# Expert products of a mixture-of-experts kernel: the high part of the weights streams both parts of its operand in one matmul

## What is computed

```python
# 1. attention with decay, block 64, q, k, v of (2, 8, 768, 64)  ->  x of (1536, 512)
# 2. mixture of experts: N, D, E, F = 1536, 512, 8, 1024
logits = x @ w_gate
expert_idx = argmax(logits, axis=1); gate_w = softmax(logits)[expert_idx]
for e in range(E):
    xe = x[expert_idx == e]
    h = maximum(xe @ w1[e], 0.0)
    out[expert_idx == e] = gate_w * (h @ w2[e])
# 3. dense: 512 -> 2048 -> 512
h = x @ w_in
y = (h - tanh(h)) @ w_out
```

## Time and profile before

| | us |
|---|---|
| median of three executions | 549.39 (548.83 to 557.4) |
| the profiled execution, its own time | 552.58 |
| its span | 550.8 |
| granted TensorE clock, mean over the span | 0.98 |
| TensorE busy, share of the span | 93% |
| experts, from the first product of the second expert to the end of the last x2_h | 118.3 to 276.2 |

### The profile page before, as it was taken

How to read it: one execution, slowest core, us unless ns; L and a number is a source line. 1 busy time by engine, 2 the same in 40 slices (tenths; PEclk the granted TensorE clock), 3 DMA queues, 4 the chain that set the end, 5 groups by cost and what they waited for, 6 DMA issues and landing times.

```text
span 550.8 us, 10819 instructions
## 1 busy us (share of the span) xinstructions
PE 511.6 (93%) x3948; PEld 454.6 (83%) x3949; DVE 364.0 (66%) x496; ACT 257.4 (47%) x467; POOL 317.8 (58%) x258
## 2 busy tenths in 40 slices
PE   2999848799999999999989999999999999999994
PEld 2899748799999999999968888888888888888883
DVE  2433275856455365454469999998998784998781
ACT  0222216556566566566454545545443434443431
POOL 4566235634454454444449889985855553875553
PEclk9999959999999999999999999999999999999998
DMA  7988615656757757667280000000100000100002
GB/s 223 374 292 281 225 31 175 205 169 208 234 175 227 230 196 222 195 210 232 90 302 6 2 0 1 0 1 20 58 0 0 1 1 1 58 20 1 1 0 77
DMA packets 33450, 65.35 MB, mean 119 GB/s; under 512 B 3680, under 2 KB 8800, under 8 KB 33376
## 3 DMA queue, kind: packets, MB, share of 16 engines
q1 hardware_dynamic: 31488, 58.49, 32.7%
q0 software_dynamic: 1920, 6.29, 3.5%
HBM read 58.22 MB, written 6.55 MB: 118 GB/s over the span
## 4 chain that ended last, share of the span: by engine, by line
PE 85%; DMA 5%; DVE 3%; issue 3%; ACT 2%; SPq 1%; POOL 1%; ACTq 0%; DVEq 0%; POOLq 0%
PE bank L306 25%; PE bank L308 24%; PE bank L307 24%; DMA wst<-in_w_dram 3%; PE bank L1075 3%; PE bank L1052 2%; PE bank L1063 2%; PE bank L1097 1%; PE bank L1087 1%; PE bank L1161 1%; PE bank L1104 1%; DVE x_sorted L952 1%; DMA w_gate_sb<-in_w_gate_dram 1%; POOL out_dram L621 1%; DMA x_sorted<-token_rows,tokid 1%
## 5 line engine op out<-in xcount | busy, mean ns | idle before, releaser
L579 POOL TENSOR_TENSOR w_l<-wst,w_h 128x512 fp32r<-128x512 f32 x64 | 84.4, 1319 | 107.4 <-ACT w_h L684 107.3
L629 POOL TENSOR_SCALAR big<-h_sq 128x512 uint8<-128x512 f32 x48 | 79.8, 1663 | 38.3 <-ACT h_sq L768 38.0
L642 POOL TENSOR_TENSOR g_l<-g,g_h 128x512 fp32r<-128x512 f32 x48 | 63.6, 1325 | 46.5 <-ACT g_h L778 46.5
L306 PE MATMUL bank<-wo_h,g_h 128*128 128x512 f32 x192 | 75.4, 393 | 0.0
L308 PE MATMUL bank<-wo_l,g_h 128*128 128x512 f32 x192 | 75.1, 391 | 0.0
L307 PE MATMUL bank<-wo_h,g_l 128*128 128x512 f32 x192 | 74.6, 389 | 0.0
L308 PE MATMUL bank<-x_l,win_h 128*128 128x512 f32 x188 | 74.4, 395 | 0.0
L306 PE MATMUL bank<-x_h,win_h 128*128 128x512 f32 x188 | 73.9, 393 | 0.0
L306 PE MATMUL bank<-xs_h,w_h 128*128 (+1 forms) x256 | 71.3, 279 | 2.6 <-DVE xs_l L958 1.4
L307 PE MATMUL bank<-x_h,win_l 128*128 128x512 f32 x188 | 73.7, 392 | 0.0
L306 PE MATMUL bank<-h_h,w_h 128*128 128x232 f32 x256 | 71.6, 280 | 1.7 <-DVE h_l L942 1.6
(11 more groups left out here) (145 smaller groups left out, 1094.7 us busy)
## 6 DMA issues: line engine op xcount, KB each, us to landing
wst<-in_w_dram SPq DMA_DIRECT2D x128, 256.0 KB, 3.0
qk_in<-in_qk_t_dram SPq DMA_DIRECT2D x12, 512.0 KB, 5.5
kv_in<-in_kv_dram SPq DMA_DIRECT2D x12, 512.0 KB, 5.2
win<-in_w_in_dram SPq DMA_DIRECT2D x8, 512.0 KB, 4.7
wo<-in_w_out_dram SPq DMA_DIRECT2D x8, 512.0 KB, 8.6
token_rows<-x_sb SPq DMA_DIRECT2D x12, 256.0 KB, 3.5
mask<-decay_powers SPq DMA_DIRECT2D x4, 128.0 KB, 3.3
decay_powers<-powers SPq DMA_DIRECT2D x1, 256.0 KB, 2.9
```

The costliest lines, as they stand in the source:

```text
L306: pe.matmul(dst, lh, rh, start=start, stop=False, skip_group_check=True)
L579: pool.tensor_tensor(w2_l[:, j % STG], wst2[:, j % STG], w2_h[:, j % 2].bitcast(F32), ALU.subtract).then_inc(w2l_ready, 1)
L629: pool.tensor_scalar(big[:, f % 2], h_sq[:, f % 2], T * T, None, ALU.is_ge).then_inc(big_ready, 1)
L642: pool.tensor_tensor(g_l[:, f % 2], g[:, f % 2], g_h[:, f % 2].bitcast(F32), ALU.subtract).then_inc(gl_ready, 1)
```

## The change

Each product makes two matmuls where it had three. The high weight part streams both parts of the operand (464 columns) into the two halves of one bank; the low weight part streams the high part of the operand (232 columns) into the first half. A bank so holds two partial results, and they are added when the bank is read out:

- `hidden`: DVE first adds the two halves (a reduction over an axis of two, from PSUM, to h_plain in SBUF, L966 of the new file); ACT takes relu of that to the high part (L700); DVE makes the low part (L969), now from two operands in SBUF. Hidden banks alternate between 0 and 1.
- y takes four banks (4 to 7) of two halves each, and there is one such set. After an expert's last product ACT copies the second halves to `rows` in two pieces (`y_in`, L728), DVE adds the first halves to them (L996) giving x2, at unit 0 of the next expert; at unit 1 `y_out` makes x2_h and x2_l from x2, now in SBUF. The second product of unit 0 of the next expert waits for the two sums.
- The turned tiles use banks 2 and 3; xs_h and xs_l become one tensor xs.

```diff
+        def both(b):
+            return bank[:, b, 0:2 * WIN].rearrange("p (a t) -> p a t", a=2)
...
+        def y_bank(half, side):
+
+            return bank[:, 4 + 2 * half:6 + 2 * half, side * WIN:(side + 1) * WIN]
+
+        def two(pe, b, lh, ll, r, start, stop):
+
+            pe.matmul(both(b), lh, r, start=start, stop=False, skip_group_check=True)
+            return pe.matmul(both(b)[:, 0], ll, r[:, 0], start=False, stop=stop, skip_group_check=True)
...
 # ACT
             def hidden(j, unit):
-                act.wait_ge(first_done, unit + 1)
-                act.activation(h_h[:, j % 2], bank[:, j % 4, 0:WIN], ACT.Relu).then_inc(hh_ready, 1)
+                act.wait_ge(hsum_ready, unit + 1)
+                act.activation(h_parts[:, j % 2, 0], h_plain[:, j % 2, 1], ACT.Relu).then_inc(hh_ready, 1)
...
+            def y_in(expert_no, off):
+
+                for half in range(2):
+                    if half:
+                        act.wait_ge(second_done, JT * expert_no)
+                    else:
+                        act.wait_ge(y_half_done, expert_no)
+                    act.copy(rows[:, 2 * half:2 * half + 2, bass.ds(off, WIN)], y_bank(half, 1)).then_inc(y_side_ready, 1)
+
+            def y_out(expert_no, off):
+                act.wait_ge(y_sum_ready, 2 * expert_no)
+                act.copy(x2_h[:, :, bass.ds(off, WIN)], x2[:, :, bass.ds(off, WIN)]).then_inc(y_high_ready, 1)
...
                     hidden(j, unit)
+                    if j == 0 and not first:
+                        y_in(e, off)
...
 # DVE
             def hidden(j, unit):
+                dve.wait_ge(first_done, unit + 1)
+                dve.tensor_reduce(h_plain[:, j % 2, 1], both(j % 2).rearrange("p a t -> p t a"), AX.X,
+                                  ALU.add).then_inc(hsum_ready, 1)
                 dve.wait_ge(hh_ready, unit + 1)
-                dve.scalar_tensor_tensor(h_l[:, j % 2], bank[:, j % 4, 0:WIN], 0.0, h_h[:, j % 2].bitcast(F32),
+                dve.scalar_tensor_tensor(h_parts[:, j % 2, 1], h_plain[:, j % 2, 1], 0.0, h_parts[:, j % 2, 0].bitcast(F32),
                                          ALU.max, ALU.subtract).then_inc(hl_ready, 1)
...
+            def y_in(expert_no, off):
+
+                for half in range(2):
+                    sl = slice(2 * half, 2 * half + 2)
+                    dve.wait_ge(y_side_ready, 2 * expert_no - 1 + half)
+                    dve.tensor_tensor(x2[:, sl, bass.ds(off, WIN)], y_bank(half, 0), rows[:, sl, bass.ds(off, WIN)],
+                                      ALU.add).then_inc(y_sum_ready, 1)
...
 # PE
-                    i = three(pe, bank[:, j % 4, 0:WIN], w1_h[:, j % 2, k, :], w1_l[:, j % STG, k, :],
-                              xs_h[:, k, bass.ds(off, WIN)], xs_l[:, k, bass.ds(off, WIN)], k == 0, k == KT - 1)
+                    i = two(pe, j % 2, w1_h[:, j % 2, k, :], w1_l[:, j % STG, k, :], xs[:, k, :, bass.ds(off, WIN)],
+                            k == 0, k == KT - 1)
...
+                    if j == 0 and k % 2 == 0 and summed is not None:
+
+                        pe.wait_ge(y_sum_ready, summed + k // 2)
                     sl = slice(k * P, (k + 1) * P)
-                    i = three(pe, psYs[side][:, k], w2_h[:, j % 2, sl], w2_l[:, j % STG, sl], h_h[:, j % 2], h_l[:, j % 2],
-                              j == 0 and k % 2 == 0, j == JT - 1)
+                    i = two(pe, 4 + k, w2_h[:, j % 2, sl], w2_l[:, j % STG, sl], h_parts[:, j % 2], j == 0, j == JT - 1)
+                    if j == JT - 1 and k == 1:
+                        i.then_inc(y_half_done, 1)
```

More of the change, by code:

```diff
@@ L118, in decay_attention_moe_kernel @@
         rows, x2_h = twice("rows", "x2_h", [P, KT, PAD])
[L119 removed]
+        x2, x2_l = twice("x2", "x2_l", [P, KT, PAD])
         win_h = sb("win_h", [P, KT, F2], F32R)
@@ L180, in decay_attention_moe_kernel @@
         expert_no = sb("expert_no", [1, E, OV], at=experts_mem)
-        h_h = sb("h_h", [P, 2, WIN], F32R, at=experts_mem)
-        h_l = sb("h_l", [P, 2, WIN], F32R, at=experts_mem)
+        h_plain, h_parts = twice("h_plain", "h_parts", [P, 2, 2, WIN], at=experts_mem)
         experts_mem.close()
@@ L594, in _, with expert @@
                 gather(t)
-            def expert(e, side, first=False, last=False):
+            def expert(e, first=False, last=False):
                 for j in range(JT):
@@ L734, in expert @@
                     if j == 1 and not first:
-                        y_out(JT * e, off, 1 - side, e - 1)
+                        y_out(e, off)
                     if j == (JT - 1 if first else 3):
@@ L983, in expert @@
                     if j == 1 and not first:
-                        y_out(e, off, 1 - side)
+                        y_out(e, off)
                     if j == (JT - 1 if first else 3):
@@ L1195, in expert @@
                         first_product(offset(e + 1), 0, JT * e + JT)
-                    if j == 0 and not first:
-                        ge(pe, y_low_ready, e - 1)
                     if first:
                         turn(LATER[j])
-                    second_product(j, JT * e + j, side)
+                    second_product(j, JT * e + j, None if first else 2 * e - 1)
             pe.wait_ge(ov_step, 2)
```

55 lines of the change are left out of this document (31 added, 24 removed).

## The result

The changed kernel takes 573.07 us (median of 4, 572.3 to 574.2), the kernel before 549.11 (median of 4, 547.0 to 557.4): a ratio of 1.0423, interval 1.038 to 1.0466. It is slower, on the side forecast and inside the range, 5.4 us above the point. Of one kernel's executions, those over 1.5% above its fastest (here the 557.4) are left out of the ratios and intervals of this document. The profiled execution took 572.8 us, 20.2 above the profiled one of before, where I had worked out 18.3.

What follows compares the result with a forecast made beforehand. Experts looked bound by TensorE, but DVE and ACT were already on the path where x2_h and x2_l are made. 9 + 4.9 + 3.7 + 0.5 = +18; 549.4 + 18.3 = 567.7 us, range 557 to 580.

Steps and rivals of the forecast that it cites:

- The two waits: In each expert TensorE idles for h_parts at units 2 and 4, behind x2_l and win_l: 1.85 and 1.3 us.
- a plain unit: A unit without output or split work: 2.58 us instead of 2.68, the hidden part's round trip hidden.
- The lock of the ports: VectorE with two SBUF inputs and GpSimd exclude each other; h_l can be held, at worst 1 us more per round trip.
- Five experts: The long stretch between second expert and last: +1.8 us an expert, +9 in all.
- first boundary: First change of expert, split of w_in still in front: 27.0 us against 22.1, +4.9.
- first expert: Expert with the turned tiles: slower steps of 3.7 to 4.1 us, offset by the incident's going; net +0.5 us.
- incident: First expert before: a scaling of 4.62 us behind POOL instructions, then a lower clock; 3.3 us lost, taken as gone.
- The last expert: Seven units, both waits, and 1.25 us more behind the last matmul: 28.2 against 24.5, +3.7.
- The dense stage: Stage after the experts: forecast as untouched by the change.
- the slow reduction: Rival: reading pairs 232 columns apart, the reduction takes 1.12 us and DVE sets the pace; 590 us, chance 0.08.
- TensorE did not stay the bound: Rival that TensorE stays the bound, waits as before: 540 to 544 us, below 538 with faster 464-column matmuls; chance 0.09.
- The incident returns: Rival: POOL's instructions again in a row as DVE scales in the first expert; 572 to 573 us, chance 0.13.

Runs made afterwards that it cites:

- no_sum: Changed kernel without DVE's reduction in the hidden part, relu and low part reading the first half of the bank alone: 548.79 us, 0.9942 of the kernel before.
- late_lows: Changed kernel with all of x2_l and win_l made behind the last expert, the reduction kept: 558.7 us (one execution), an expert 20.93 us.
- pieces: Changed kernel with x2_h, x2_l, win_h and win_l made in four pieces each, spread over units, behind the reduction: 549.42 us, 0.9981 of the kernel before.
- sum_first: Changed kernel with the reductions of units 2 and 4 put ahead of x2_l and win_l: 571.18 us, 1.0393 of the kernel before.
- before_pieces: Kernel before, three matmuls kept, with x2 copies and win splits in four pieces each: 548.34 us, 0.9952 of the kernel before.
- pieces_hoist: As pieces, plus in the first expert the next unit's reduction ahead of the turned tiles' low parts: 547.22 us, 0.9954 of the kernel before.
- sum_first_split: As sum_first, with POOL making w2_l in two instructions of 256 columns: 569.2 us, 1.0305 of the kernel before.
- sum_first_u2: Changed kernel with only the reduction of unit 2 put ahead of x2_l: 571.48 us, 1.0387 of the kernel before.
- pieces_hoist_split: As pieces_hoist, with POOL making w2_l in two instructions of 256 columns: 548.5 us, 0.9976 of the kernel before.

## Why the prediction was right, and where it was off

**Right in the mechanism.** DVE between product and relu, and behind it the low part of x2 and the split of w_in: `no_sum` gives back all of the slowdown, and `late_lows` and `pieces` show that the reduction costs nothing where no long step stands ahead of it. The two waits measured 1.65 and 1.32 in the expert shown, 1.54 to 1.89 and 1.27 to 1.31 in the other experts of the long stretch, as far as they have a row, 1.54 and 1.55 in the second expert (forecast 1.85 and 1.3), a plain unit 2.57 (2.58), the reduction 0.63 (0.64), a 464-column matmul 0.21. An expert took 24.29 against 24.1. The lock of the ports, which I let fall on h_l, met x2_l instead: 1.45 us where I had 1.12.

**The terms.** Five experts +10.1 for +9; first boundary +5.4 for +4.9, with TensorE waiting 2.35 for the sums as worked out (2.4) and 0.32 for the last hidden part (1.0); first expert −0.3 for +0.5, the steps between turns 3.65 to 4.47 where I had 3.7 to 4.1, and no incident. It is gone in this trace and in those of `sum_first`, `late_lows`, `pieces` and `before_pieces`, but since the kernel before itself has it in different sizes, and `pieces_hoist` has it again, my reason (POOL is not in a row any more in that order) was not tested.

Some sums do not come out as written. The four terms make 18.1, and 18.3 went into the time. The first boundary takes the two waits at 1.3 and 1.3 where the walk had 1.85 and 1.3. For the last expert, 1.8 an expert and 1.25 behind it make 3.05, not 3.7. For the first, 4.6 and 0.6 less 3.3 is +1.9, less the 1.8 for the clock too +0.1; neither is +0.5. None of this is over 1.5 us.

**The last expert, +3.7 forecast, +4.7 to x2_h ready.** I counted a copy, one sum and x2_h, 2.1 us, behind the last matmul. The chain has 3.2 from 292.97, where half of y is there, or some 2.6 from the end of the last matmul at about 293.5: both sums follow the copy, 0.61 and 0.65 one behind the other, and the handovers come to 0.35. Two more waits of TensorE were not in the forecast: 0.36 for the second sum of the expert before, and 0.39 for the last unit's own round trip (290.40 to 292.05), which has no next first product to hide it.

**The dense stage, "untouched" in the forecast, cost +1.5.** TensorE was idle 2.69 us ahead of it; then 12 matmuls ran at a granted clock of 0.69 and the first two behind them took 0.43, not 0.23. That the hole could cost clock as well I had seen in the incident of the earlier trace rows and not applied here. Whether that is the change's doing stays open: before, a hole of 2.41 us was followed by a full clock in the first trace, while the second one, behind a hole of 2.12, had 4.47 us for the same 12 matmuls. The gap of 1.35 us that did not return, −1.2, was in no term either; that the two nearly cancel is luck.

**What put the point 5.4 us low is mostly the base.** I said "I add the difference to the median": 549.4 + 18.3. But the difference was made against a trace that holds the incident at 4.62 us, and I counted its going as a gain, while the median execution lies 3.2 under that trace. The base should have been the profiled execution: 552.6 + 18.3 = 570.9, within 2.2 of the result. So 3.2 of the 5.4 us come from the base, 1.9 from the terms, and 0.3 from a median of the changed kernel that lies above its own trace. The median of before looks low too: 59 later executions of that kernel, in three groups, have medians of 550.0 to 551.5. The traces show the incident changing from run to run; that it is what lifts that one execution above the median is argued, not shown.

**Of the rivals,** the slow reduction fell (464 elements, read in pairs 232 apart, 0.63 on the line of steps that read PSUM side by side). TensorE did not stay the bound. "The incident returns" gave a number near the result (572 to 573) by the wrong mechanism: in the trace of 572.8 us every scaling took 0.48 or 0.49.

## What to carry to other kernels

A shorter instruction on the busiest engine gains only what the others leave it: here a pair that saved 0.1 us a unit put one more step on DVE between two products, and each long step queued on DVE ahead of it became a wait of 1.3 to 1.9 us. Before making such a change, look at what stands in the queue ahead of the new step; cut it into pieces that fit the place where the engine waits anyway, or spread them over the units. Such pieces alone, without the pair, gave the kernel before the same 0.5%.

Taking a result from PSUM into SBUF first can lengthen the step that reads it next: x2_l went from 1.12 to 1.45 us beside POOL.

If a trace holds a stall that may not be in every execution, keep that trace's own time as the base for a forecast that takes the stall away, and take a second trace of the same kernel first.

## What the runs showed of the hardware

- DVE's h_parts, two inputs in SBUF, took 0.40 alone and 1.50 beside one POOL instruction of 1.26 us (`sum_first`); 0.91 beside POOL instructions half as wide. Halving POOL's instructions cut the single hold, from 1.10 to 0.52, but not the sum of the holds in a unit (`sum_first_split`).
- The same subtraction of 128x928, x2_l, took 1.12 in 8 of 8 cases with one input in PSUM (`before`), and with both in SBUF 1.44 to 1.46 in the seven cases beside POOL, 1.13 in the one without (the changed kernel).
- The same scaling of 128x512 on DVE took 0.48, 1.72, 1.81, 3.92, 4.62 or 4.80 us in different traces; 1.81 and 4.62 are the same kernel. The one of 4.62 us, 102.42 to 107.04, ran beside POOL instructions that stood end to end from 102.63 to 106.75.
- After 2.1 to 2.7 us without TensorE work, the next 12 matmuls of 512 columns took 3.02 or 3.03 us at the full clock in three traces (`before`, `no_sum`, `before_pieces`), and 4.17 to 5.46 us in nine others; the granted clock over their first 4.1 us was 0.68 in the changed kernel and 0.50 in the two slowest (`sum_first_u2`, `pieces_hoist_split`). One kernel, `before`, shows both.
- A float32 matmul of 464 columns takes 0.21 from its start to the next one's, one of 232 columns 0.11: beside the 0.11 for 128 columns, a pair of one wide and one narrow takes 0.32 where three narrow ones take 0.335. From 232 upwards, in these rows, the time goes by the columns (696 in both groups) and hardly by the number of matmuls.
